# Scores in quarters of TensorE's array and the gate's weights in strips of 32 columns, in a fused attention and mixture-of-experts kernel

## The reference

```python
# q, k, v: 4 batches, 8 heads, 576 positions, 64 columns
scores = scale * np.matmul(q, k.transpose(0, 1, 3, 2))
mask = (rel >= 0) & (rel < 128)
scores = np.where(mask, scores + bias[None], -1e9)
attn = softmax(scores)
x = np.matmul(attn, v)            # regrouped to 2304 tokens x 512
logits = x @ w_gate               # 8 experts
# greedy by descending logit: each token one expert, each expert 288 tokens
out[mask] = np.maximum(x[mask] @ w1[e], 0.0) @ w2[e]
h = out @ w_in
return (h / (1 + np.exp(-h))) @ w_out
```

## Time and profile before

| | us |
|---|---|
| median of 3 runs | 860.61 |
| the profiled execution | 861.91 |
| its span | 860.2 |
| TensorE busy | 827.4 |
| VectorE busy | 494.5 |
| ScalarE busy | 330.3 |
| GpSimd busy | 306.7 |

### The profile page before, as it was taken

One profiled execution on the slowest core, in us unless ns is written; L12 is line 12 of the kernel. 1 busy time (PEld: TensorE's weight loads), 2 busy tenths in 40 slices (PEclk: granted clock), 3 DMA queues, 4 the chain that ended last, 5 costly groups with the idle time before them and its releaser, 6 DMA issues.

```text
span 860.2 us, 17129 instructions
## 1 busy us (share of the span) xinstructions
PE 827.4 (96%) x6459; PEld 773.0 (90%) x6459; DVE 494.5 (57%) x1590; ACT 330.3 (38%) x767; POOL 306.7 (36%) x336
## 2 busy tenths in 40 slices
PE   5999999937999999999999999999999999999997
PEld 5999999926988998999899888998998899899996
DVE  7778787665855666475655443756556566542111
ACT  3655566513323432433343224333432433343221
POOL 1443333502435323523433235234332623433223
PEclk9999999957999999999999999999999999999999
DMA  9887888305104303230430040404301240431000
GB/s 148 179 169 160 174 165 172 103 14 171 54 1 126 111 13 98 67 86 2 126 106 18 1 126 13 123 2 126 99 26 45 83 123 2 127 88 36 1 1 37
DMA packets 154626, 71.39 MB, mean 83 GB/s; under 512 B 98992, under 2 KB 140976, under 8 KB 154544
## 3 DMA queue, kind: packets, MB, share of 16 engines
q1 hardware_dynamic: 149200, 60.56, 28.7%
q0 software_dynamic: 2976, 9.44, 3.6%
q10 hardware_dynamic: 2368, 0.30, 0.3%
HBM read 60.83 MB, written 9.44 MB: 82 GB/s over the span
## 4 chain that ended last, share of the span: by engine, by line
PE 74%; DVE 3%; POOL 1%; issue 1%; DMA 1%; ACT 0%; SPq 0%; POOLq 0%; DVEq 0%
PE hp L1127 12%; PE hp L1128 11%; PE hp L1129 11%; PE acc L1212 8%; PE acc L1214 8%; PE acc L1213 8%; PE acc L1127 4%; PE acc L1129 4%; PE acc L1128 4%; PE rt L1079 2%; DVE test L1379 1%; DMA wa_raw<-in_moe_w_dram 1%; PE rt L1094 0%; DVE test L1375 0%; PE acc L1121 0%
## 5 line engine op out<-in xcount | busy, mean ns | idle before, releaser
L1055 POOL TENSOR_TENSOR h_l<-h_raw,h_h 128x256 fp32r<-128x256 f32 (+1 forms) x128 | 115.5, 903 | 265.5 <-ACT h_h L1336 265.3
L1605 DVE TENSOR_TENSOR h_raw<-hp,gate 128x256 f32<-128x256 f32 (+1 forms) x128 | 58.5, 457 | 179.9 <-ACT gate L1328 179.0
L1127 PE MATMUL hp<-xy_h,res_h 128*128 128x256 f32 (+1 forms) x512 | 154.0, 301 | 0.0
L1128 PE MATMUL hp<-xy_l,res_h 128*128 128x256 f32 (+1 forms) x512 | 151.4, 296 | 0.0
L1129 PE MATMUL hp<-xy_h,res_l 128*128 128x256 f32 (+1 forms) x512 | 151.2, 295 | 0.0
L1043 POOL TENSOR_TENSOR wb_l<-wb_raw,wb_h 128x512 fp32r<-128x512 f32 x64 | 86.6, 1354 | 125.6 <-ACT wb_h L1272 125.5
L1328 ACT ACTIVATE gate<-hp 128x256 f32<-128x256 f32 (+1 forms) x128 | 52.6, 411 | 195.4 <-PE hp L1129 193.7
L1212 PE MATMUL acc<-res_h,h_h 128*128 128x512 f32 x288 | 116.7, 405 | 0.0
L1214 PE MATMUL acc<-res_h,h_l 128*128 128x512 f32 x288 | 113.5, 394 | 0.0
L1213 PE MATMUL acc<-res_l,h_h 128*128 128x512 f32 x288 | 113.5, 394 | 0.0
L1127 PEld LDWEIGHTS hp<-xy_h,res_h 128*128 128x128 f32 x512 | 96.5, 188 | 3.6
(11 more groups left out here) (216 smaller groups left out, 1684.3 us busy)
## 6 DMA issues: line engine op xcount, KB each, us to landing
wa_raw<-in_moe_w_dram SPq DMA_DIRECT2D x64, 256.0 KB, 3.3
wb_raw<-in_moe_w_dram SPq DMA_DIRECT2D x64, 256.0 KB, 3.0
k_rows<-in_k_dram SPq DMA_DIRECT2D x64, 72.0 KB, 3.7
q_rows<-in_q_dram SPq DMA_DIRECT2D x60, 72.0 KB, 2.7
v_rows<-in_v_dram SPq DMA_DIRECT2D x32, 128.0 KB, 2.5
stage<-in_moe_w_in_dram SPq DMA_DIRECT2D x8, 512.0 KB, 4.6
x_rows<-x_rows_sb SPq DMA_DIRECT2D x16, 256.0 KB, 4.2
stage<-in_moe_w_out_dram SPq DMA_DIRECT2D x8, 512.0 KB, 4.3
```

The lines of the kernel that those rows point to most:

```text
L1055: pool.tensor_tensor(h_l[:, cols], h_raw[:, cols], h_h[:, cols].bitcast(FP32), ALU.subtract).then_inc(g_low, 1)
L1127: nc.tensor.matmul(out_, weights_h, cols_h, start=start, stop=False)
L1128: nc.tensor.matmul(out_, weights_h, cols_l, start=False, stop=False)
L1605: nc.vector.tensor_tensor(h_raw[:, h_cols(s, f)], hp[(A_NO[s, f] - 1) % 2][:, 0:width], gate[:, 0:width], ALU.mult).then_inc(g_done, 1)
```

## The change

Scores. `qT` loses its zeros and its second copy of columns. Each unit becomes two products, one for each head, with 64 rows and 64 columns of stationary operand, placed on a quarter of the array: an even unit takes the quarters (0, 0) and (64, 64), an odd one (0, 64) and (64, 0). Even and odd units write to banks of their own, so `s_ps` has four banks, and `t_ps` and `m_ps` have one each. On odd units the heads change sides; the bias is held for both sides, and `turn_probs` writes the heads back in order.

Gate. The weights of the gate, padded from 8 to 32 columns, become stationary on one strip of 32 columns of the array, and the turned rows of x are moved past them. The first four tiles of 128 tokens go to four strips; the fifth tile (64 tokens) goes to each of the four. The result has experts as rows; it is taken up in `grown` by VectorE once for each pair, in spare columns of `o_ps[0]`, and once per batch two transposes and two copies bring it to `logits`.

Moves. The last tile of x is turned in the slot of kind 3, its copy and the gate come in the slot of kind 0 behind it. q is turned in one instruction. The bias of pairs 1 to 3 is made in slots 0, 4 and 8.

```diff
-        s_ps, t_ps, o_ps, m_ps = pb("s_ps"), pb("t_ps"), pb("o_ps"), pb("m_ps")
+        s_ps = [pb("s_even"), pb("s_odd")]
+        t_ps, o_ps, m_ps = pb("t_ps", 1)[0], pb("o_ps"), pb("m_ps", 1)[0]
+
+        x_banks = [(m_ps, m_ps)] * (NG - 1) + [(s_ps[0][1], s_ps[1][1])]
...
+            def gate_logits(g):
+
+                if g == 0:
+                    pe.wait_ge(wg_loaded, 16)
+                    pe.wait_ge(wg_padded, 1)
+                pe.wait_ge(x_taken, g + 1)
+                pe.wait_ge(e_taken, g + 1)
+
+                pe.wait_ge(norm_done, TILES_TO[min(4 * (g + 2) - 1, NS)])
+                for t, strip in [(t, t) for t in range(TB - 1)] + [(TB - 1, strip) for strip in range(TB - 1)]:
+
+                    at = slice(STRIP * strip, STRIP * (strip + 1))
+                    o = LT_COL + P * (t // (TB - 1))
+                    last = nc.tensor.matmul(o_ps[0][at, o:o + ROWS[t]], wg[:, g % PAIRS, :], xT[:, P * t:P * t + ROWS[t]],
+                                            start=True, stop=True, tile_position=(0, STRIP * strip))
+                last.then_inc(lg_done, 1)
+
+            def turn_logits(b):
+
+                pe.wait_ge(lg_copied, PAIRS * (b + 1))
+                nc.tensor.transpose(m_ps[:, 0:P], grown[:, 0:P], ident[:])
+                nc.tensor.transpose(m_ps[0:TAIL, P:P + STRIP], grown[0:STRIP, P:P + TAIL],
+                                    ident[0:STRIP, 0:STRIP]).then_inc(lg_turned, 1)
...
-                    last = nc.tensor.matmul(s_ps[s % 2][:, c:c + kw], qT[g % 2][:, u, :], kT[g % 2][:, k0:k0 + kw],
-                                            start=True, stop=True)
+                    c = bank_col(u)
+                    for h in range(2):
+
+                        at, side = slice(U * h, U * (h + 1)), h ^ (u % 2)
+                        to = slice(U * side, U * (side + 1))
+                        last = nc.tensor.matmul(s_ps[u % 2][s % 2][to, c:c + kw], qT[g % 2][at, U * u:U * (u + 1)],
+                                                kT[g % 2][at, k0:k0 + kw], start=True, stop=True,
+                                                tile_position=(U * h, U * side))
...
-                if s >= 2:
-                    pe.wait_ge(pT_ready, s - 1)
+                if s >= 1:
+                    pe.wait_ge(pT_ready, s)
...
-                    turn_x_end(g - 1)
-                if kind == 3 and g >= 1:
-                    gate_logits(g - 1, slice(0, TB))
+                if kind == 0 and g >= 2:
+                    gate_logits(g - 2)
+                if kind == 1 and g >= PAIRS + 1 and g % PAIRS == 1:
+                    turn_logits(g // PAIRS - 1)
             turn_x_main(NG - 1)
             weighted_values(NS - 1)
-            pe.wait_ge(lg_added, NG - 1)
-            gate_logits(NG - 1, slice(0, main_tiles(NG - 1)))
             turn_x_end(NG - 1)
-            gate_logits(NG - 1, slice(main_tiles(NG - 1), TB))
+            gate_logits(NG - 1)
+            turn_logits(B - 1)
...
-                at = slice(U * h, U * (h + 1))
-                nc.vector.transpose(qT[g % 2][at, :, at],
-                                    q_rows[g % RING_IN][at].rearrange("p n d -> p (n d)").rearrange("p (u m) -> p u m", m=U)
-                                    ).then_inc(q_turned, 1)
-
-            def add_logits(g):
-
-                b = g // PAIRS
+                nc.vector.transpose(qT[g % 2][:], q_rows[g % RING_IN][:].rearrange("p n d -> p (n d)")).then_inc(q_turned, 1)
+
+            def take_grown(g):
+
+                b, pair = divmod(g, PAIRS)
                 dve.wait_ge(lg_done, g + 1)
-                if g >= 1:
-                    dve.wait_ge(lg_added, g)
+                made = o_ps[0][:, LT_COL:LT_COL + P + TAIL]
+                if pair == 0:
+                    if b >= 1:
+                        dve.wait_ge(lg_turned, b)
+                    nc.vector.tensor_copy(grown[:], made).then_inc(lg_copied, 1)
                 else:
+                    dve.wait_ge(lg_copied, g)
+                    nc.vector.tensor_tensor(grown[:], made, grown[:], ALU.add).then_inc(lg_copied, 1)
+
+            def take_logits(b):
+
+                dve.wait_ge(lg_turned, b + 1)
...
+                nc.vector.tensor_copy(logits[:, TB * b:TB * b + TB - 1, :],
+                                      m_ps[:, 0:P].rearrange("p (t e) -> p t e", e=STRIP)[:, :, 0:E])
+                nc.vector.tensor_copy(logits[0:TAIL, TB * b + TB - 1, :], m_ps[0:TAIL, P:P + E]).then_inc(lg_added, 1)
...
-            nc.vector.memset(qT[0][0:U, :, U:P], 0.0)
-            nc.vector.memset(qT[0][U:P, :, 0:U], 0.0)
...
+            for side in range(2):
+                dve.wait_ge(pool_seq, 1)
+                at = slice(U * side, U * (side + 1))
+                for parity in range(2):
+                    nc.vector.tensor_scalar(steep[at, parity, :], rel[at, :], -float(U) * side,
+                                            -(D ** 0.5) * 2.0 ** (-8.0 * ((side ^ parity) + 1) / H), ALU.add, ALU.mult
+                                            ).then_inc(steep_ready, 1)
...
+            def make_bias(pair):
+
+                nc.vector.scalar_tensor_tensor(bias[:, pair], steep[:], 2.0 ** (-16.0 * pair / H),
+                                               masked[:, None, :].to_broadcast([P, 2, KEYS]), ALU.mult, ALU.add
+                                               ).then_inc(bias_ready, 1)
```

More of the change, by code:

```diff
@@ L190, in main_tiles @@
     return TB - 1 if g + 1 < NG else TB - 2
-def logits_at(g):
-    return P * (TB - main_tiles(g))
+STRIP = 32
+LT_COL = 4 * (D + 1)
 SQ = 32
@@ L222, in attention @@
         v_rows = [sb(f"v_rows{i}", [P, TB, 2, D + 1]) for i in range(RING_IN)]
-        qT = [sb(f"qT{i}", [P, UNITS, P]) for i in range(2)]
+        qT = [sb(f"qT{i}", [P, S]) for i in range(2)]
         kT = [sb(f"kT{i}", [P, S]) for i in range(2)]
@@ L406, in turn_x_end @@
                 c = slice(P * (g % PAIRS), P * (g % PAIRS + 1))
[L407 to L408 removed]
+                pe.wait_ge(x_taken, g + 1)
                 pe.wait_ge(norm_done, tiles_of_pair(g))
                 for n, t in enumerate(range(main_tiles(g), TB)):
[L411 removed]
+                    last = nc.tensor.transpose(x_banks[g][1][:, P * n:P * (n + 1)], x_rows[:, t, c], ident[:])
                 last.then_inc(e_turned, 1)
[L414 to L422, removed]
[L423 to L426 removed]
+            def gate_logits(g):
+                if g == 0:
+                    pe.wait_ge(wg_loaded, 16)
+                    pe.wait_ge(wg_padded, 1)
+                pe.wait_ge(x_taken, g + 1)
+                pe.wait_ge(e_taken, g + 1)
[11 more added lines that the diff above has]
+                                    ident[0:STRIP, 0:STRIP]).then_inc(lg_turned, 1)
             def scores(s):
@@ L454, in turn_probs @@
                     region, parity = divmod(n, 2)
-                    to = t_ps[s % 2][:, 2 * P * region:2 * P * (region + 1)].rearrange("p (h u m) -> p h u m", h=2, u=2)
-                    last = nc.tensor.transpose(to[:, :, parity, :], from_, ident[:])
+                    to = t_ps[:, 2 * P * region:2 * P * (region + 1)].rearrange("p (h u m) -> p h u m", h=2, u=2)
+                    to = to[:, ::-1 if parity and (s % 4 or region) else 1, parity, :]
+                    last = nc.tensor.transpose(to, from_, ident[:])
                 last.then_inc(t_done, 1)
@@ L465, in weighted_values @@
                     pe.wait_ge(norm_done, TILES_TO[s - 1])
+                if s % 4 == 0 and s >= 8:
+                    pe.wait_ge(lg_copied, s // 4 - 1)
                 for n, (g, t) in enumerate(slot_tiles(s)):
@@ L556, in _ @@
                     copy_x(g - 1)
-                    copy_x_end(g - 1)
+                if kind == 0 and g >= 2:
+                    copy_x_end(g - 2)
                 if s + 1 < NS:
@@ L702, in _ @@
             bias_and_max(1)
-            turn_q(1, 0)
+            turn_q(1)
             for s in range(NS):
                 g, kind = divmod(s, 4)
-                if kind == 0 and g >= 2:
-                    add_logits(g - 2)
                 if s + 2 < NS:
+                    if kind == 2 and 1 <= g + 1 < PAIRS:
+                        dve.wait_ge(bias_ready, g + 2)
                     bias_and_max(s + 2)
+                if kind == 0 and g + 1 < PAIRS:
+                    make_bias(g + 1)
                 if s >= 1:
@@ L714, in _ @@
                 if kind == 3 and g + 2 < NG:
-                    turn_q(g + 2, 0)
-                if kind == 0 and g + 1 < NG:
-                    turn_q(g + 1, 1)
-                if kind >= 1 and g >= PAIRS + 1 and g % PAIRS == 1:
-                    rank_batch(g // PAIRS - 1, kind - 1)
+                    turn_q(g + 2)
+                if kind == 0 and g >= 2:
+                    take_grown(g - 2)
+                if g >= PAIRS + 1 and g % PAIRS == 1:
+                    if kind == 1:
+                        take_logits(g // PAIRS - 1)
+                    elif kind > 1:
```

(6 more changed lines are left out.)

76 lines of the change are left out of this document (32 added, 44 removed).

## The result

| | before | changed |
|---|---|---|
| first comparison, median (lowest to highest) | 860.6 us (860.46 to 862.47, 4 runs) | 891.65 us (867.71 to 915.77, 4 runs) |
| ratio, 95% interval | | 1.0081, 1.0065 to 1.0097 |
| second comparison, median (lowest to highest) | 861.48 us (860.55 to 862.37, 18 runs) | 863.32 us (855.45 to 937.43, 13 runs) |
| ratio, 95% interval | | 0.9987, 0.9965 to 1.0009 |
| the profiled execution, its span | 861.91, 860.2 us | 867.71, 865.9 us |

The ratios compare only the faster runs of each kernel, and what they leave out here is not a disturbance but the change itself: the kernel before never left 860 to 863 us, and 17 runs of the changed one lie between 855 and 937, their middle one at 864.

A forecast was written before the change was run, and what follows sets the result against it. Only TensorE was taken to bind attention. Scores +9.0, gate -5.2, mode changes +10.7, start -0.5 and end +1.5 made +15.5 on 861.9, 877.4; with the median 1.3 lower, 876 us, range 839 to 898.

The forecast's parts named there:

- the case I held likeliest: Scores and gate on TensorE: records overlap in pairs only; 862 to 890 us, chance 0.42.
- Quarters in pairs only: Scores: a product's second record runs only beside the next product's first; 0.82 us a slot against 0.65, in all +9.0 us.
- The first rival: Scores and gate: all four quarters run together, loads set the pace, -12.5 and -9.8 us; 839 to 860 us, chance 0.31.
- Change between whole array and tiles: TensorE, around scores and gate: each switch of array mode bares 0.074 us, 144 switches, +10.7 us.
- Rows taken up at no cost: Values waiting for `take_grown`: 1.1 us of scores and transposes cover about 0.6 us of addition, so nothing.
- The third rival: TensorE gets faster, but the single bank or VectorE holds a pair near 9.5 us; 852 to 857 us, chance 0.07.
- One bank for the turned probabilities: `turn_probs` waits for the previous slot's copy; costs nothing, with 0.5 us of cover.
- Loads: DMA issue on SyncE's queue: unchanged but for the counts, costing nothing.
- Start and end: First scores at about 7.7 us, start term -0.5 us; gate, addition, transposes and copies before ranking, end term +1.5 us.
- The clock: TensorE's granted clock stays 1.00 from about 15 us to attention's end; if lower, every term is too small; no size given.

The follow-up runs named there:

- scores_only: The changed kernel with the gate's arithmetic of before (ten records, added to the logits per pair); median 864.6 us, 860.0 to 887.1 in 12 runs.
- gate_only_m: gate_only with the gate's rows in m_ps[1] instead of o_ps[0], so the values don't wait for VectorE; median 856.8 us, ratio 0.9941.
- warmfill_m: warmfill with the gate's rows written to m_ps instead of the spare columns of o_ps[0]; median 856.2 us, ratio 0.9941.
- m_load: fill_m_load without its ten added whole-array products; median 862.6 us, 851.0 to 913.5 in 12 runs, ratio 0.9938.
- a0_again: The changed kernel run again, unchanged; median 863.3 us, 855.5 to 937.4 in 13 runs, ratio 0.9987.
- fill_m_load: fill_m with SyncE issuing the loads of the pair three ahead before the staging load and stores; median 854.5 us, ratio 0.9924.
- warm16: The changed kernel with 16 whole-array products on TensorE before the first scores; median 865.0 us, 854.3 to 883.8, ratio 0.9951.
- fill_m: fill_only with the gate's rows written to m_ps instead of o_ps[0]; median 856.8 us, 855.0 to 872.7, ratio 0.9935.
- before_gap: The kernel before, with the third block of scores held until VectorE has taken the second; median 863.9 us, ratio 1.0032.
- gate_only: The kernel before with only the gate's part of the change, scores and banks kept; median 868.2 us, ratio 1.0069.
- warmfill: The changed kernel with 16 whole-array products before the first scores and 19 in the first slots; median 862.2 us, ratio 1.0010.
- fill_only: The changed kernel with 2 whole-array products in each of slots 1 to 5, none ahead of the first scores; median 856.8 us, ratio 0.9953.

## Why the prediction was right or wrong

The forecast was 876.0, +15.5 us on the profiled execution. The ratio says +0.8%, 7 us, and the second comparison says none. The range of 839 to 898 holds both medians, and the sign of the first comparison is that of the forecast. Both are luck: where it is slower, the cause is one that none of my cases had, and the case I held likeliest is refuted. At the upper clock a pair takes 9.22 us and not 11.0.

*Quarters in pairs only: wrong.* "Nothing in the trace shows a record overtaking another" was an argument from absence, and it failed. Four first records start within 20 ns, then the four second ones: a slot block takes 0.49 us, where I had 0.82 plus 0.074. The first rival had 0.43 plus 0.074 = 0.50. The pair gave -0.28 (scores_only), the rival -0.19, my forecast +1.2 with its mode changes. The gate's block, 0.47 against 1.08 (rival: 0.43), gave -0.50 (gate_only_m) with its change of mode. One of the rival's own terms was added up wrongly: 0.64 against 0.82 in a slot of kind 0 is -0.18 and not -0.12, so its scores come to -13.4 and the rival about 1 us lower. The page of the Trainium skill that I set against my choice was the better guide here. "TensorE: Matmul & The Clock Gate", Part 3, has small tiles start some 4 ns apart, and here they start 5 to 8 ns apart. Whether the chip or the program's layout puts the second records behind the others', the trace doesn't tell.

*Change between whole array and tiles: right.* I took 0.074 us. The first gate record comes 0.93 behind the first of eight values (98.19 to 99.12), where eight values cost 0.85: 0.08. From the last wave of scores to the transposes it is 0.26 (95.41 to 95.67), against a stream of 0.163: 0.10. The Trainium skill's "TensorEngine Tiling (Array Packing)", section Tiling Modes, is borne out in kind, at a half to two thirds of the 0.148 that a full drain would have bared.

*Rows taken up at no cost: wrong.* My cover of 1.1 us against 0.6 counted the addition and not what stands ahead of it on VectorE, nor that the block of scores in that cover would itself shrink. Alone it cost 0.55 us a pair and, at two of the batch ends, 2.1 us with a fall of the clock behind it. In the changed kernel it is part of the pairs of 9.4 to 10.2 us. The third rival had waits take over, but by the single bank or by VectorE's total, and not by this one; and its 852 to 857 are counted from the profiled execution, from the median they would be 851 to 856.

*One bank for the turned probabilities: right*, nearly. Only 0.2 us before one transpose at attention's end (173.65) is laid to it in the changed kernel. Where k comes late it is more: 2.2 us in seven waits in warmfill_m. *Loads: missed.* I wrote that SyncE's queue was unchanged. Its work is, but a pair is 0.9 us shorter and k came late. That the one comes of the other is likely and not shown.

*Start and end.* The first scores came at 8.44 us, not 7.7, but the first transpose of probabilities comes 2.0 us earlier than before, where the term was -0.5. From the last division to ranking it takes 3.4 us instead of 2.0 (181.23 - 177.82 against 175.51 - 173.47): +1.4, where I had +1.5.

*The clock: missed, though named.* I wrote that a lower granted clock would make the prediction wrong in a way that none of the rivals holds, and gave it no mechanism, price or chance. It is the largest term. One pair at the lower level costs 16.1 - 9.2 = 6.9 us, so the first three pairs alone (12.83, 16.09 and 11.86 us here; 9.30, 8.76 and 9.22 in the profile of m_load) hold 13.5 us of this execution. In a0_again, at 884.9, the same excess is 24.5 us in the first four pairs and 5 more in the last, behind the fall. That later rises and falls also make the times up to 937 is an inference, because no run above 885 has a profile. The step that failed was to put the clock's term at nothing: I read the earlier trace rows, where the clock is 1.00, as a property of the stage. It belonged to the stream that I was about to change.

What stays open is by what property the stream with quarters keeps a low clock from rising, and why it does so in some runs only. The runs show that the scores' part of the change is enough and that the gate's part isn't needed, that a pause of 0.8 us alone on whole-array scores doesn't do it, and that ten whole-array products at the start cure it, be it as whole-array work or by filling the pause. The steps of about 9 us in the times of scores_only weren't explained either. Whether fill_m_load keeps its clock in every run of a larger number wasn't tried beyond six.

## What to carry to other kernels

Work in tiles of the array can speed up a stage bound by TensorE and yet lose its clock: here a pair fell from 10.11 to 9.22 us, and the runs spread over 82. Read the clock from the distances of equal records in the first microseconds, not from the busy line, and look at the spread of many runs before a median. If the clock has to be won at the start of such a stage, try a little whole-array work until it is up, and then keep long pauses away. When a stage gets shorter, recheck each engine that was "unchanged": its queue has less time for the same work.

## What the hardware showed that I had not expected

- At the lower clock TensorE stayed busy for 39.93 of 40 us (warm16) and 36.00 of 36 us (fill_m), both on streams with quarters, without the clock rising. On streams with whole-array scores it rose at 15.1 to 15.5 us in the profiles of before, before_gap and gate_only, at 14.7 in that of gate_only_m, and came back in 6.8 and 3.4 us after falls (gate_only). With quarters in the scores and nothing added at the start it rose at 16.1, 16.5, 45.4 and 69.9 us, and after falls it came back in 41.0 (warm16), 37.5 (fill_m), 17.1 (warmfill) and 13.7 us (a0_again).
- Each of the six falls inside attention came in or up to 2.4 us behind a pause in which TensorE waited for VectorE: 1.83 us (warm16), 2.09 and 2.07 (gate_only), 1.40 (warmfill), 1.21 (fill_m) and 1.09 (a0_again). Pauses of 1.33 us (fill_only, to 109.36) and 1.03 (warm16, to 124.98) had no fall behind them.
- Eight fp32 records on four quarters run in two waves of four. The second wave starts 0.21 us behind the first, 0.05 more than the 0.163 of a whole-array record of 192 columns. The block takes 0.49 us with the way back to the whole array, without the 0.1 or so of the way in, against 0.65 for four whole-array records of the same work.
- The gate's 16 records on strips start 5 to 8 ns apart within a wave, and take 0.47 us where ten records with 128-column loads took 1.08.
